# Retention and two mixtures of experts: where chunk sums are kept, which engine splits them, and what the loads wait for

## The reference

```python
for t in range(S):                                   # retention
    state = gamma * state + outer(k[t], v[t])
    y[t] = scale * q[t] @ state
logits = x @ w_gate; P = exp(logits - logits.max())  # first mixture: 8 experts
for _ in range(8):
    P /= P.sum(1) + 1e-9; P /= P.sum(0) + 1e-9; P *= N / E
out += P[:, e] * (relu(x @ w1[e]) @ w2[e])           # w1: 512 x 1024, w2: 1024 x 512
p = domain_probs / (domain_probs.sum(-1) + 1e-9)     # second mixture: 4 experts
out += p[:, e] * (relu(x @ w1[e]) @ w2[e])
```

## Time and profile before

| | us |
|---|---|
| median of 3 runs | 1548.74 (1548.64 to 1549.47) |
| the profiled execution's own time | 1548.59 |
| its span, first to last instruction | 1546.8 |
| TensorE busy | 1538.3 |
| VectorE, ScalarE, GpSimd busy | 882.2, 441.6, 55.0 |

### The profile page before, as it was taken

One profiled execution on the slowest core, in us unless ns is written; L12 is line 12 of the kernel. 1 busy time (PEld: TensorE's weight loads), 2 busy tenths in 40 slices (PEclk: granted clock), 3 DMA queues, 4 the chain that ended last, 5 costly groups with the idle time before them and its releaser, 6 DMA issues.

```text
span 1546.8 us, 21387 instructions
## 1 busy us (share of the span) xinstructions
PE 1538.3 (99%) x8312; PEld 1395.1 (90%) x8312; DVE 882.2 (57%) x1419; ACT 441.6 (29%) x840; POOL 55.0 (4%) x45
## 2 busy tenths in 40 slices
PE   8999999999999999999999999999999999999999
PEld 7889988998899889988998899889998999899988
DVE  8656855555546545555464455576555556455553
ACT  4422321322223213222232132243331223213311
POOL 6200000000000000000000000012000000000000
PEclk9999999999999999999999999999999999999999
DMA  9100101101001011010010110101101001011011
GB/s 347 57 28 28 55 1 55 42 14 55 26 29 54 0 54 39 16 54 24 30 54 0 54 40 16 55 1 56 55 1 55 28 28 54 0 54 55 1 43 67
DMA packets 34602, 66.62 MB, mean 43 GB/s; under 512 B 2032, under 2 KB 2672, under 8 KB 34544
## 3 DMA queue, kind: packets, MB, share of 16 engines
q1 hardware_dynamic: 34112, 65.63, 12.2%
q10 hardware_dynamic: 432, 0.18, 0.0%
HBM read 62.66 MB, written 3.15 MB: 43 GB/s over the span
## 4 chain that ended last, share of the span: by engine, by line
PE 98%; DVE 1%; DMA 1%; issue 0%; SPq 0%; DVEq 0%
PE banks L1151 17%; PE banks L1152 17%; PE banks L1150 17%; PE banks L1129 15%; PE banks L1133 15%; PE banks L1131 15%; PE banks L1007 1%; DMA qt_in<-in_q_t 0%; PE banks L1042 0%; PE banks L1093 0%; PE banks L1037 0%; DMA small<-in_c_small 0%; DVE scores L637 0%; PE banks L1026 0%; PE banks L1073 0%; PE banks L1075 0%
## 5 line engine op out<-in xcount | busy, mean ns | idle before, releaser
L1129 PE MATMUL banks<-x_hi,w_hi 128*128 128x384 f32 x1344 | 449.9, 335 | 1.4 <-DVE w_lo L665 1.3
L1133 PE MATMUL banks<-x_hi,w_lo 128*128 128x384 f32 x1344 | 449.5, 334 | 0.0
L1131 PE MATMUL banks<-x_lo,w_hi 128*128 128x384 f32 x1344 | 449.3, 334 | 0.0
L1152 PE MATMUL banks<-w_hi,h_lo 128*128 128x512 f32 x1148 | 447.6, 390 | 0.0
L1151 PE MATMUL banks<-w_lo,h_hi 128*128 128x512 f32 x1148 | 447.4, 390 | 0.0
L1150 PE MATMUL banks<-w_hi,h_hi 128*128 128x512 f32 x1148 | 446.9, 389 | 0.0
L866 DVE SCALAR_TENSOR_TENSOR acc<-banks,gate,acc 128x512 f32<-128x512 f32 x251 | 188.5, 751 | 372.5 <-PE banks L1152 372.5
L540 ACT COPY ups<-banks 128x384 f32<-128x384 f32 x288 | 138.1, 480 | 900.5 <-PE banks L1133 900.3
L818 DVE TENSOR_TENSOR ups<-banks,ups 128x384 f32<-128x384 f32 x288 | 155.5, 555 | 190.2 <-ACT ups L540 168.4
L1129 PEld LDWEIGHTS banks<-x_hi,w_hi 128*128 128x128 f32 x1344 | 252.4, 188 | 4.0 <-DVE w_lo L665 2.0
L1152 PEld LDWEIGHTS banks<-w_hi,h_lo 128*128 128x128 f32 x1148 | 215.4, 188 | 44.9
(11 more groups left out here) (100 smaller groups left out, 492.9 us busy)
## 6 DMA issues: line engine op xcount, KB each, us to landing
w_raw<-in_moe_w SPq DMA_DIRECT2D x46, 1024.0 KB, 5.0
kt_in<-in_k_t SPq DMA_DIRECT2D x12, 256.0 KB, 4.3
qt_in<-in_q_t SPq DMA_DIRECT2D x12, 256.0 KB, 5.7
v_in<-in_v SPq DMA_DIRECT2D x12, 256.0 KB, 5.9
k_in<-in_k SPq DMA_DIRECT2D x10, 256.0 KB, 5.8
out<-acc SPq DMA_DIRECT2D x2, 768.0 KB, 3.5
out<-acc SPq DMA_DIRECT2D x5, 256.0 KB, 2.0
w_raw<-in_moe_w SPq DMA_DIRECT2D x4, 256.0 KB, 6.3
```

The lines of the kernel that those rows point to most:

```text
L1129: nc.tensor.matmul(o, w1_hi[:, w, kc, fs], x_hi[:, x, kc, at], start=start and kc == 0, stop=False, skip_group_check=True)
L1131: nc.tensor.matmul(o, w1_hi[:, w, kc, fs], x_lo[:, x, kc, at], start=False, stop=False, skip_group_check=True)
L1133: last = nc.tensor.matmul(o, w1_lo[:, w, kc, fs], x_hi[:, x, kc, at], start=False, stop=kc == 1, skip_group_check=True)
L1152: last = nc.tensor.matmul(o, h_lo[:, f, b, rows], w2_hi[:, f, :], start=False, stop=(n == UC - 1))
```

## The change

The four sums and B12 of a chunk go to a tile x_whole of the shape of x_lo, declared in a scope that is closed again ahead of x_lo, so that both have the same place in SBUF; a chunk's low parts then overwrite its sums. x_raw and its waits go. SyncE waits per load. Score(1) gets bank 6 for its second half and no wait. powers are made first for the heads, then, behind mask(0), for the rises. GpSimd takes the low parts of the sums of chunks 3, 4 and 5 and those of w2_first. VectorE's first low part of w1 comes ahead of chunk 4's sums. The two halves of the logits are taken apart: the first stays, the second comes behind the third group of the first down.

```diff
+        with ExitStack() as whole:
+            x_whole = sb("x_whole", [P, 7, 2, SEQ], F32, whole)
...
+        def x_sums_at(n):
+
+            return x_whole[:, X_T1:X_T4 + 1, :, x_at(n)]
+
+        def b12_at(n):
+            return x_whole[:, X_B22, :, x_at(n)]
+
         def score_bank(s, r):
-            return bank[(2 * s + r) % 3]
+
+            return bank[6] if (s, r) == (1, 1) else bank[(2 * s + r) % 3]
...
 
+                    sp.wait_ge(scored, 2 * (s - 4) + 2)
+                if c > 2:
+                    sp.wait_ge(q_raised, s - 4 - BATCH + 1)
+                load_qk(c, b)
+                if c < CH - 1:
+                    if c > 1:
+                        sp.wait_ge(k_decayed, s - 4 + 1)
+                    load_k(c, b)
+                if c > 1:
                     sp.wait_ge(y_done, s - 4 + 1)
-                load_qk(c, b)
-                load_kv(c, b)
+                load_v(c, b)
...
             def sums_low(n):
                 pool.wait_ge(x_hit, n + 1)
-                nc.gpsimd.tensor_tensor(x_lo[:, X_T1:X_T4 + 1, :, x_at(n)], x_sum,
+
+                pool.wait_ge(x_lot, n)
+                nc.gpsimd.tensor_tensor(x_lo[:, X_T1:X_T4 + 1, :, x_at(n)], x_sums_at(n),
...
+            def first_w2_low():
+                for g in range(2):
+                    at = slice(2 * g, 2 * g + 2)
+                    pool.wait_ge(w2_hi_ready, g + 1)
+                    nc.gpsimd.tensor_tensor(w2_lo[:, at, :], w2_first[:, at, :], w2_hi[:, at, :].bitcast(F32),
+                                            ALU.subtract).then_inc(w2_ready, 1)
...
-            sums_low(CH - 1)
+            first_w2_low()
+            for n in range(CPB, CH):
+                sums_low(n)
...
-                if n > 0:
-
-                    act.wait_ge(x_summed, n)
-                nc.scalar.copy(b12, x_banks(n)[:, 0:2 * P].rearrange("p (k t) -> p k t", k=2)).then_inc(x_b12, 1)
+                nc.scalar.copy(b12_at(n), x_banks(n)[:, 0:2 * P].rearrange("p (k t) -> p k t", k=2)).then_inc(x_b12, 1)
...
-                if b == 0 and c > 0:
+                if b == 0 and 0 < c < CH - 1:
...
-                    sums_high(CH - 1)
+                    act.wait_ge(w2_in, 16)
+                    for g in range(2):
+                        at = slice(2 * g, 2 * g + 2)
+                        nc.scalar.copy(w2_hi[:, at, :], w2_first[:, at, :]).then_inc(w2_hi_ready, 1)
+                    sums_high(CH - 2)
                 if x2 is not None:
                     x2_high(x2)
                 for half in range(2):
                     hidden_copy(k, p, 3, half, U_U4)
-                if first:
-                    act.wait_ge(w2_in, 16)
-                    for g in range(2):
-                        at = slice(2 * g, 2 * g + 2)
-                        nc.scalar.copy(w2_hi[:, at, :], w2_first[:, at, :]).then_inc(w2_hi_ready, 1)
                 for half in range(2):
                     act.wait_ge(summed, sums_before(k, p) + (half + 1))
                     hidden_high(2 + half, 1, ups[:, half, U_U4, :])
                     act.wait_ge(up_done, ups_before(k, p) + (2 * 4 + half + 1))
                     hidden_high(half, 1, up_psum(ON_X, half))
+                if first:
+                    sums_high(CH - 1)
...
-                if n > 0:
-
-                    dve.wait_ge(x_lot, n)
...
+                sums = x_sums_at(n)
+                then_wait(nc.vector.tensor_tensor(sums[:, 0, :, :], b12_at(n), b11, ALU.subtract))
+
+                then_wait(nc.vector.tensor_tensor(sums[:, 1:3, :, :], b22.unsqueeze(1).to_broadcast([P, 2, 2, P]),
+                                                  x_whole[:, X_B22:X_T1 + 1, :, x_at(n)], ALU.subtract))
+                nc.vector.tensor_tensor(sums[:, 3, :, :], b21, sums[:, 2, :, :], ALU.subtract).then_inc(x_summed, 1)
 
             def x_low(n):
-                dve.wait_ge(x_hib, n + 1)
+
+                dve.wait_ge(x_summed, n + 1)
...
-            for b in range(BATCH):
-                nc.vector.memset(state[b][:, :, :], 0.0).then_inc(zeroed, 1)
+
+            nc.vector.memset(state[1][:, 0:2, :], 0.0).then_inc(zeroed, 1)
...
+            def powers_of(groups):
+                n_groups = groups.stop - groups.start
+                then_wait(nc.vector.tensor_copy(powers[:, groups, 0:LOADED],
+                                                power_steps[:, 0:LOADED, groups].rearrange("p w g -> p g w")))
+                for n in range(DOUBLINGS):
+                    w = LOADED << n
+                    factor = power_steps[:, LOADED + n, groups].unsqueeze(2).to_broadcast([P, n_groups, w])
+                    made = nc.vector.tensor_tensor(powers[:, groups, w:2 * w], powers[:, groups, 0:w], factor, ALU.mult)
+                    if n < DOUBLINGS - 1:
+                        then_wait(made)
+                return made
+
+            then_wait(powers_of(slice(0, HEADS)))
             dve.wait_ge(causal_in, 16)
             then_wait(nc.vector.tensor_tensor(powers[:, 0:HEADS, :], powers[:, 0:HEADS, :],
                                               causal[:, :].unsqueeze(1).to_broadcast([P, HEADS, P]), ALU.mult))
             mask_scores(0)
+            powers_of(slice(HEADS, HEADS + DC)).then_inc(rise_made, 1)
...
-                if b == 0 and c > 0:
+                if b == 0 and 0 < c < CH - 1:
                     x_sums(c - 1)
+                if b == 1 and 0 < c < CH - 1:
+                    x_low(c - 1)
+                if s in (5, 7, 9):
+                    sums_low((s - 5) // 2)
                 if s == STEPS - 2:
                     first_w1_low(0)
-                if s == STEPS - 1:
-                    first_w1_low(1)
-                    first_w1_low(2)
-                if b == 1 and c > 0:
-                    x_low(c - 1)
-                    sums_low(c - 1)
-            x_low(CH - 1)
-            x_sums(CH - 1)
+            first_w1_low(1)
+            first_w1_low(2)
+            x_sums(CH - 2)
+            x_low(CH - 2)
             split_w1_low(0, 2)
             split_w1_low(0, 3)
 
@@ -831,7 +848,8 @@
                     dve.wait_ge(copied, copies_before(k, p) + (4 + half + 1))
                     hidden_sum(k, p, half, half, U_U4, ON_Y)
                 if first:
-                    first_w2_low()
+                    x_sums(CH - 1)
+                    x_low(CH - 1)
...
-                if s > 0:
+                if s > 1:
...
-            def logits():
-
-                pe.wait_ge(wg_lo_ready, 1)
-                x_split(CH)
+            def logits(p):
+                if p == 0:
+                    pe.wait_ge(wg_lo_ready, 1)
+                else:
+                    x_split(CH)
+
+                    pe.wait_ge(h_ready, 4)
+                at = slice(p * BLK, (p + 1) * BLK)
...
+                    if first and u == 2:
+                        logits(1)
...
-            logits()
+
+            x_read(CH - 1)
+            logits(0)
 
             pe.wait_ge(logits_out, 1)
             down(0, 0, first=True)
```

More of the change, by code:

```diff
@@ L91, in retention_moe_moe_kernel @@
         w2_lo = sb("w2_lo", [P, UC, DM], F32R)
-        x_raw = sb("x_raw", [P, 5, 2, P])
-        b12, x_sum = x_raw[:, 0, :, :], x_raw[:, 1:5, :, :]
         ident = sb("ident", [P, P])
@@ L292, in load_w2 @@
                 sp.dma_start(to, src).then_inc(w2_in, 16)
[L294 to L297, removed]
             load_qk(0, 0)
@@ L450, in sums_high @@
                 act.wait_ge(x_summed, n + 1)
-                nc.scalar.copy(x_hi[:, X_T1:X_T4 + 1, :, x_at(n)], x_sum).then_inc(x_hit, 1)
+                nc.scalar.copy(x_hi[:, X_T1:X_T4 + 1, :, x_at(n)], x_sums_at(n)).then_inc(x_hit, 1)
             def state_out(s, b):
@@ L660, in sums_low @@
                 dve.wait_ge(x_hit, n + 1)
-                low(x_lo[:, X_T1:X_T4 + 1, :, x_at(n)], x_sum,
+                low(x_lo[:, X_T1:X_T4 + 1, :, x_at(n)], x_sums_at(n),
                     x_hi[:, X_T1:X_T4 + 1, :, x_at(n)]).then_inc(x_lot, 1)
@@ L710, in split_w1_low @@
                         w1_hi[:, at, :, :].rearrange("p m k f -> p k m f")).then_inc(w1_ready, 1)
[L712 to L716, removed]
             def split_w2(k):
@@ L1049, in warm @@
                     nc.tensor.matmul(bank[7][:, 0:P], state[1][:, 0:2, :], state[1][:, 0:2, :], start=True, stop=True)
-            pe.wait_ge(zeroed, 4)
+            pe.wait_ge(zeroed, 3)
             warm(WARM)
@@ L1058, in _ @@
                 attend(s)
-            def logits():
-                pe.wait_ge(wg_lo_ready, 1)
-                x_split(CH)
-                parts = [(0, X_B11, 64), (2, X_B21, P), (0, X_T1, 0), (2, X_B22, 0)]
-                for p in range(PAIRS):
-                    if p == 1:
-                        pe.wait_ge(h_ready, 4)
-                    for n, (c, m, w) in enumerate(parts):
-                        for kc in range(2):
-                            at = slice(p * BLK, (p + 1) * BLK)
```

(17 more changed lines are left out.)

4 lines of the change are left out of this document (removed).

## The result

| | before | after |
|---|---|---|
| median us (7 runs each) | 1548.74 | 1553.88 |
| profiled execution, its span | 1548.59, 1546.8 | 1554.29, 1552.5 |

The ratio is 1.0033 with a 95% interval of 1.0022 to 1.0045: 5.1 us slower. The forecast was 2.1 us slower than the profiled execution of before (1550.7), with 1552.8 as the upper end of its range; the mechanism that it gave is there, and on top of it came the rival called "the clock falls in the new gap".

A forecast was written before the change was run, and what follows sets the result against it. TensorE, busy 1538.3 of 1546.8 us, was taken as the bound. Having won 2.3 us up to logits(0), the first unit loses it: 69.15 against 67.05, so 1548.59 + 2.1 = 1550.7 us; range 1546.8 to 1552.8.

The forecast's parts named there:

- the mechanism that it gave: First unit: GpSimd holds VectorE, delaying ScalarE's relu and logits copy; TensorE idles 4.4 us before the first down product.
- the clock falls in the new gap: Rival, 15%: after the 4.4 us gap ahead of the first down product, matmuls run at half rate; 1552.5 us.
- the hold: First unit: GpSimd's SBUF operations make VectorE's hidden_low 0, 2 and 4 wait; first down product starts at 66.4 us.
- The clock's price: Half-rate matmuls behind the gap cost 1 to 2 us, read from the first matmuls; 1.8 in the rival's sum.
- the clock's own case: The forecast plus 1.8 us for half-rate matmuls behind the gap: 1552.5 us, chance 15%.
- Loads: Attention: q requested 2 to 3 us sooner removes TensorE's longer waits ahead of scores 7 to 9; 0.45 us won.
- The start: Up to score(2): it starts at 11.85 instead of 12.00 us; 0.15 us won, bounds -0.1 and +0.2.
- The tail of attention: From score(11), at 39.87, to the first up product, at 44.2 us: that product starts 2.3 us sooner (1.5 to 2.6).
- Product 4: First up: it can start at 52.91 us, after ScalarE's copy of product 3, where it wanted 52.86.

The follow-up runs named there:

- experiment 4: Changed kernel with SyncE's old waits put back (y of four steps ago ahead of all four loads of a step); 1554.34 us.
- experiment 6: Changed kernel with the low parts of the first w2 back on VectorE, ahead of chunk 5's sums; 1555.72 us.
- experiment 3: Changed kernel with 22 unused matmuls of 384 columns behind the first half of the logits, filling most of TensorE's gap; 1551.95 us.
- experiment 1: Changed kernel with ScalarE's copy of the logits' first half moved ahead of its last four relus of the first unit; 1548.48 us.
- experiment 2: Changed kernel, GpSimd holding the low parts of chunks 3 to 5's sums until VectorE wrote all eight hidden low parts; 1548.52 us.
- experiment 7: Experiment 1's kernel with SyncE's old waits put back; 1548.77 us.
- experiment 11: Kernel before, with only the waits of the loads changed to the finer ones; 1548.79 us against 1548.67.
- experiment 10: Kernel before, with only the start changed (score(1)'s second half in bank 6 without its wait, heads' powers first); 1548.81 us against 1548.67.
- experiment 5: Changed kernel with the second half of the logits again directly behind the first, ahead of the first down product; 1549.15 us.
- experiment 8: Changed kernel with the early logits copy, logits' first half in bank 7, GpSimd's sums' low parts after four hidden low parts; 1550.17 us.
- experiment 9: Changed kernel, logits' first half in bank 7, second half behind the fourth group, GpSimd's sums' low parts after eight hidden low parts; 1548.22 us.
- experiment 12: Experiment 9's kernel with ScalarE's high parts of the first w2 again behind its copies of product 3's result; 1547.51 us against 1548.43.

## Why the prediction was wrong

The path was right and two terms of the sum were not. The forecast of 1550.7 us lacks 0.5 us for the loads' gain that did not come (the down product is at 66.93, not at 66.4) and 2.95 us for the clock, which its sum had at nothing: 1550.7 + 0.5 + 2.95 = 1554.15, and the profiled execution took 1554.29.

- **The clock.** The step that failed is to leave the fall of the clock out of the sum, as a rival of 0.15 beside the forecast's 0.45. With the hold it was not a rival but its consequence: a gap of 4.4 us was predicted, 4.2 came, and the clock fell behind it. It also did in the profiles of experiments 4 and 6, with gaps of 4.3 and 4.6, and in none of the others, where TensorE's longest idle time behind its first matmul was 0.8 to 2.3 us. Experiment 3 shows the cause: with work in the gap the clock stays. The trace of before had no idle time between matmuls above 1.91 us to tell it, and the page of the Trainium skill cited there (TensorE: Matmul & The Clock Gate, Part 1) spoke for it. Of the 18 executions of the three kernels with the gap (the changed one, 4 and 6), 17 show a clock below full and one, in experiment 4, does not: it should have had the larger share, if not all.
- **The clock's price** was put at 1.8; it measured 2.95 from the starts, 2.85 by experiment 3, and 2.3 and 2.5 in experiments 4 and 6. It was scaled from the warm-up, where 3 us ran at half rate; after the gaps 4.8 to 6.1 us did. With this price in it the range would just have reached the result; as it stood, even the clock's own case ended too low, at 1552.5.
- **The hold** was right in place, order and size: hidden_low 0 and 2 held, the down product at 66.9 instead of 66.4. Experiments 1 and 2 show it. The rule of the Trainium skill (SBUF — State Buffer, Who interferes with whom) gave the right direction again in experiment 6, against what the change looks like.
- **Loads** (0.45, bounds 0.1 and 0.45): no gain that can be told, by experiments 7 and 11. The waits for q went, and TensorE's unexplained stops and a longer wait for q(4) came in their place. From score(2) to score(11) 28.0 us were forecast and 29.15 came (28.5 before): 1.1 us too much, against which the start stood at 0.55 better than forecast. That leaves the 0.6 by which the first up product was late (44.80, not 44.2).
- **The start** (0.15, bounds up to 0.2): 0.7 in the changed kernel's profile, but nothing in experiment 10. It varies from one execution to the next by more than the term, with the engine that is first at the first meeting.
- **The tail of attention** was right: from score(11) to the first up product 4.34 us, predicted 4.33 (44.2 - 39.87), before 6.04.
- **Product 4** was reckoned at 0.05 us of wait; it holds where w2_first is in time, and is about 1.0 us in four profiles (5, 6, 8 and 9).

## What to carry to other kernels

When a ledger of waits ends in a gap of TensorE longer than any in the trace, count the matmuls behind it at half rate as part of the forecast, not as an accident; here gaps of 4.2 us and more did it, at 2.3 to 3 us each, and gaps of up to 2.3 us did not. An operation of GpSimd that reads SBUF costs VectorE up to nearly its own length when VectorE needs two inputs from SBUF (here up to 1.7 us for one of 2.4), so it belongs where VectorE reads PSUM or rests; and before two pieces of TensorE's work are taken apart, ask which copy the second one was hiding.

## What the runs showed of the hardware that was not expected

TensorE stopped for 0.2 to 0.4 us inside a row of matmuls of one score, for nothing that the profile shows, at the same places in nine profiles, only with loads requested earlier. The 1 MB load of w2_first landed at 50.2 to 50.7 us in seven profiles (before, after, experiments 1, 2, 3, 7, 12), at 51.2 and 51.3 in two (4, 11) and at 51.8 to 52.6 in five (5, 6, 8, 9, 10). The requests lie between 44.9 and 46.2 us; from request to landing the load took 5.1 to 5.5 us in the first nine and 6.3 to 6.8 in the last five; why, no run shows. Where VectorE's causal product and GpSimd's k_dec(0) meet, the one that starts first keeps its time and the other waits it out, even with a lead of 0.01 to 0.04 us (after: 1.23 and 2.12 us; experiment 11: 2.08 and 1.04), and which it is moves the start of this kernel by some tenths.
